# Gates in the gathered rows, and a first mixture that adds its results into a zeroed table

## What is computed

```python
x = _attn_ref(**attn_kwargs).reshape(B * S, D)
# first mixture: logits + log1p(exp(x @ w_noise)) * noise, the two best, softmax over the two
for e in range(E):
    for k in range(2):
        mask = top2[:, k] == e
        h = np.maximum(x[mask] @ w1[e], 0.0)
        out[mask] += top2_w[mask, k, None] * (h @ w2[e])
# second mixture
xn = x / (np.linalg.norm(x, axis=-1, keepdims=True) + 1e-06)
logits = xn @ en.T / tau
expert_idx = np.argmax(logits, axis=1)
gate_w = probs[np.arange(N), expert_idx]
for e in range(E):
    mask = expert_idx == e
    h = np.maximum(x[mask] @ w1[e], 0.0)
    out[mask] = gate_w[mask, None] * (h @ w2[e])
```

## Time and profile before

| | us |
|---|---|
| median of 3 runs | 1224.87 (1224.33 to 1225.34) |
| the profiled execution | 1223.82 |
| its span in the profile | 1222.1 |
| PE busy in the span | 1095.9 |

### The profile page before, as it was taken

How to read it: one execution, slowest core, us unless ns; L and a number is a source line. 1 busy time by engine, 2 the same in 40 slices (tenths; PEclk the granted TensorE clock), 3 DMA queues, 4 the chain that set the end, 5 groups by cost and what they waited for, 6 DMA issues and landing times.

```text
span 1222.1 us, 27227 instructions
## 1 busy us (share of the span) xinstructions
PE 1095.9 (90%) x8052; PEld 1039.5 (85%) x8052; DVE 744.1 (61%) x1406; ACT 553.1 (45%) x1552; POOL 523.2 (43%) x639
## 2 busy tenths in 40 slices
PE   1989188999999999999999999786389999999997
PEld 0556176999999999999999999765279999999997
DVE  8998795446464644646455465386854664466663
ACT  2222285445454544545444454355644554455552
POOL 5887002444444444444444444400324444444444
PEclk9999589999999999999999999988589999999999
DMA  9111201213131121313113111182622313124521
GB/s 325 70 63 52 73 1 42 77 42 99 39 101 42 55 83 40 98 40 101 43 39 93 39 41 41 38 268 92 240 62 64 98 42 100 39 65 125 138 61 35
DMA packets 51188, 97.89 MB, mean 80 GB/s; under 512 B 9651, under 2 KB 33051, under 8 KB 50876
## 3 DMA queue, kind: packets, MB, share of 16 engines
q1 hardware_dynamic: 33084, 61.77, 16.7%
q0 software_dynamic: 18048, 35.42, 10.1%
HBM read 69.62 MB, written 29.10 MB: 81 GB/s over the span
## 4 chain that ended last, share of the span: by engine, by line
PE 78%; DVE 12%; issue 3%; POOL 3%; ACT 2%; DMA 2%; DVEq 0%; POOLq 0%; ACTq 0%; SPq 0%
PE banks L624 22%; PE banks L626 11%; PE banks L610 9%; PE banks L616 7%; PE banks L615 7%; PE banks L611 7%; PE banks L612 7%; DVE prods L889 3%; POOL prods L443 2%; PE banks L586 2%; PE banks L594 2%; PE banks L595 2%; PE banks L550 1%; DVE choices L1092 1%; PE banks L540 1%
## 5 line engine op out<-in xcount | busy, mean ns | idle before, releaser
L1050 DVE SCALAR_TENSOR_TENSOR h_lo<-banks,h_hi 128x256 fp32r<-128x256 f32 x736 | 312.1, 424 | 372.4 <-ACT h_hi L774 315.0
L774 ACT ACTIVATE h_hi<-banks 128x256 fp32r<-128x256 f32 x736 | 283.3, 385 | 448.7 <-PE banks L616 347.6
L624 PE MATMUL banks<-w_hl,h_hi 128*128 128x384 f32 x1472 | 466.0, 353 | 0.0
L626 PE MATMUL banks<-w_hl,h_lo 128*128 128x192 f32 x1472 | 371.1, 252 | 0.0
L626 PEld LDWEIGHTS banks<-w_hl,h_lo 128*128 128x128 f32 x1472 | 279.6, 190 | 0.0
L624 PEld LDWEIGHTS banks<-w_hl,h_hi 128*128 128x128 f32 x1472 | 276.0, 188 | 0.4
L451 POOL DMA_INDIRECT x_slots<-token_rows,gather_idx x192 | 192.4, 1002 | 105.4 <-POOL gather_idx L448 76.2
L610 PE MATMUL banks<-x_hi_a,w_hi 128*128 (+1 forms) x736 | 225.0, 306 | 1.8 <-DVE x_hl_b L1018 1.7
L611 PE MATMUL banks<-x_hi_a,w_lo 128*128 (+1 forms) x736 | 206.5, 281 | 0.0
L616 PE MATMUL banks<-x_hl_b,w_lo 128*128 (+1 forms) x736 | 206.3, 280 | 0.0
L615 PE MATMUL banks<-x_hl_b,w_hi 128*128 (+1 forms) x736 | 205.8, 280 | 0.0
(11 more groups left out here) (170 smaller groups left out, 1255.3 us busy)
## 6 DMA issues: line engine op xcount, KB each, us to landing
raw<-in_moe_w SPq DMA_DIRECT2D x17, 768.0 KB
choices<-choice_rows SPq DMA_DIRECT2D x28, 384.0 KB, 4.2
raw<-in_moe_w SPq DMA_DIRECT2D x17, 512.0 KB
raw<-in_moe_w SPq DMA_DIRECT2D x34, 256.0 KB
x_halo<-in_x SPq DMA_DIRECT2D x2, 2688.0 KB, 15.1
token_rows<-stage SPq DMA_DIRECT2D x14, 384.0 KB, 2.3
token_rows<-rows SPq DMA_DIRECT2D x14, 384.0 KB, 3.9
x_slots<-token_rows,gather_idx POOLq DMA_INDIRECT x192
```

Source lines behind the costliest of these rows:

```text
L624: mm(y[:, i, 0:2 * D], h_hi[:, c % HBUFS, t], w2_hl[u][:, c, :, :], start=c == 0, stop=False)
L626: ins = mm(y[:, i, 0:D], h_lo[:, c % HBUFS, t], w2_hl[u][:, c, 0, :], start=False, stop=c == FC - 1)
L774: sc.activation(h_hi[:, c % HBUFS, :], banks[:, c % HBANKS, 0:BLOCK], ACT.Relu).then_inc(h_hi_ready[m], 1)
L1050: v.scalar_tensor_tensor(h_lo[:, c % HBUFS, :], banks[:, c % HBANKS, 0:BLOCK], 0.0, h_hi[:, c % HBUFS, :].bitcast(F32), ALU.max, ALU.subtr ...
```

## The change

Rows in memory are 193 numbers wide, the last one the gate of the row (`ROW`). Each attention group is stored twice, once for either choice, and the four gate columns follow from SP when the pair gates are ready (`store_gates`). A gather brings the gate along; POOL copies it into a ring of four blocks (`gate_ring`), and ACT and DVE scale the block's results by it, each 128-row half by itself (`take_half`, `add_half`). The first mixture's scatters add into `token_rows[1]`, which SP has filled with zeros from a piece of `logits` during attention; padding slots are added to 256 spare rows. Between the mixtures SP loads each group once, DVE sums the squares, PE turns and scores without filler products between groups. The scaling of rows by the second gate and their store are gone; two gate columns are stored instead. In `positions` the block table is made after the last one-hot, the totals come from differences of the running sum, `not_after` replaces `before` so that the subtraction of the counts is gone, and the gates are finished inside the one-hot loop. The temperature is folded into the embeddings. SP loads the second expert of the second mixture during the first. At the end of a mixture the last block is stored in halves.

```diff
+            sp.wait_ge(zeros_ready, 1)
+            zeros = logits[:, ZEROS_AT:, :].rearrange("p t e -> p (t e)")[:, 0:ROW].unsqueeze(1)
+            all_rows = token_rows[1].rearrange("(p j) d -> p j d", p=P)
+            sp.dma_start(all_rows, zeros.to_broadcast([P, (N + DUMP_ROWS) // P, ROW])).then_inc(x1_zeroed, 16)
...
-                sp.wait_ge(rows_ready[0], g + 1)
-                sp.dma_start(token_view(token_rows[0])[b, :, jj * GROUP:(jj + 1) * GROUP, :],
-                             stage[g % 2][:]).then_inc(rows_stored[g % 2], 16)
-
-
-            with sp.Fori(1, E) as e:
+                sp.wait_ge(rows_ready, g + 1)
+                for k in range(CHOICES[0]):
+                    sp.dma_start(token_view(token_rows[0][k * N:(k + 1) * N])[b, :, jj * GROUP:(jj + 1) * GROUP, 0:D],
+                                 stage[g % 2][:]).then_inc(rows_stored[g % 2], 16)
+
+            def store_gates(m):
+                for k in range(CHOICES[m]):
+                    for b in range(B):
+                        sp.dma_start(token_view(token_rows[m][k * N:(k + 1) * N])[b, :, :, D:D + 1],
+                                     gate[k][:, b * J:(b + 1) * J].unsqueeze(2), allow_slow_non_contiguous=True).then_inc(gates_stored[m], 16)
...
+            sp.wait_ge(weights_ready, 1)
+            load_expert(w1, w2, 1)
+            sp.wait_ge(gates_ready[0], 1)
+            store_gates(0)
...
+            sp.wait_ge(weights_ready, E + 1)
+            load_expert(v1, v2, 1)
...
-                sp.wait_ge(choices_used, g + 1)
...
-                                 src[b, :, jj * GROUP:(jj + 1) * GROUP, :]).then_inc(choices_in[g % CHOICE_BUFS][k], 16)
...
+                sp.dma_start(rows[:, g * GROUP:(g + 1) * GROUP, :],
+                             token_view(token_rows[1][0:N])[b, :, jj * GROUP:(jj + 1) * GROUP, 0:D]).then_inc(x1_in[g], 16)
+            sp.wait_ge(gates_ready[1], 1)
+            store_gates(1)
...
+                def take_gates(n):
+                    at = n % RING * HALVES
+                    gp.tensor_copy(gate_ring[:, bass.ds(at if isinstance(n, int) else pool.snap(at), HALVES)].unsqueeze(2),
+                                   x_slots[:, :, D:D + 1]).then_inc(gates_taken[m], 1)
...
+                    take_gates(g + 2)
...
+                    pool.wait_ge(gates_taken[m], g + 3)
...
+                        if m == 0:
+                            ins = gp.indirect_dma_start(token_rows[1], at, y_slots[:, u, i, :], None, compute_op=ALU.add)
+                        else:
+                            ins = gp.indirect_dma_start(out, at, y_slots[:, u, i, 0:D], None, bounds_check=N - 1, oob_is_err=False)
+                        ins.then_inc(stored[m], 16)
...
+                        pool.wait_ge(stored[m], g * 32)
+                        pool.sem_inc(y_slots_free[m], 1)
+                        copy_idx()
...
+                        pool.wait_ge(half_ready[m], 1)
+                        store_half(0)
+                        pool.wait_ge(y_ready[m], g + 3)
+                        pool.sem_inc(pool_tick, 1)
+                        store_half(1)
...
-            for g in range(SCALE_ACT, NG):
...
-                                 gate[0][:, tiles].unsqueeze(2).to_broadcast([P, GROUP, D]), ALU.mult).then_inc(pool_gated, 1)
...
+            mixture(0, [(rows_stored[u], 32 * (NG // 2)) for u in range(2)] + [(gates_stored[0], 16 * B * CHOICES[0])])
+            mixture(1, [(gates_stored[1], 16 * B)])
...
-            pe.wait_ge(choices_in[0][0], 16)
-            keep_clock(9)
+            keep_clock(26)
...
-                keep_clock(4)
...
+                    if i == 0:
+                        act.wait_ge(gates_taken[m], g + 1)
...
+                    if last and i == 0:
+                        act.wait_ge(half_done[m], 1)
+                    else:
+                        act.wait_ge(h_used[m], g * FC + (FC + HBUFS))
+                    sc.activation(y_half(parity(act, g), i), y[:, i, D:2 * D], ACT.Copy,
+                                  scale=slot_gate(act, g, i)).then_inc(y_copied[m], 1)
...
+                weigh()
...
-                step(v.tensor_tensor(cum[:], cum[:], counts[:], ALU.subtract))
+                step(v.tensor_tensor_scan(cum[:, 1:], flat, flat, 0.0, ALU.add, ALU.max))
+                first_of_expert, last_of_expert = cum[:, 0:E * T:T], cum[:, T::T]
+                step(v.tensor_tensor(totals[:], last_of_expert, first_of_expert, ALU.subtract))
...
+                step(v.scalar_tensor_tensor(pad_off[:], block_end[:, 0:E], float(BLOCK), first_of_expert, ALU.mult, ALU.subtract))
...
+                    if g == HOT_BUFS:
+                        finish_gates()
...
+                block_table()
...
-                v.tensor_scalar(gather_rows[:, 0:cols], q["id_tok"], 0.0, None, ALU.max).then_inc(ids_ready[m], 1)
-                step(v.tensor_scalar(q["id_pad"], ids, 0.0, float(PAD_ROW), ALU.is_equal, ALU.mult))
+                v.tensor_scalar(gather_rows[:, 0:cols], row, -1.0, 0.0, ALU.add, ALU.max).then_inc(ids_ready[m], 1)
...
-                    dve.wait_ge(y_copied[m], g + 1)
-                    slots = y_half(parity(dve, g))
-                    v.tensor_tensor(slots, y[:, :, 0:D], slots, ALU.add).then_inc(y_ready[m], 1)
+                    dve.wait_ge(y_copied[m], g * HALVES + (HALVES + i + 1))
+                    slots = y_half(parity(dve, g), i)
+                    ins = v.scalar_tensor_tensor(slots, y[:, i, 0:D], slot_gate(dve, g, i), slots, ALU.mult, ALU.add)
...
+            def weigh_pairs():
+                v.tensor_tensor(gate[1][:], best[1][:], best[0][:], ALU.subtract).then_inc(route_ask[0], 1)
+
+            def finish_pairs():
+                dve.wait_ge(route_act[0], 3)
+                step(v.tensor_scalar(gate_sum[:], gate[1][:], 1.0, 1e-9, ALU.add, ALU.add))
+                step(v.reciprocal(gate[0][:], gate_sum[:]))
+                v.tensor_tensor(gate[1][:], gate[1][:], gate[0][:], ALU.mult).then_inc(gates_ready[0], 1)
+
+            positions(0, weigh_pairs, finish_pairs)
...
-                    part = choices[u][:, k, :].rearrange("p (i d) -> p i d", d=D)
-                    v.tensor_tensor(part, part, gate[k][:, bass.ds(g * GROUP, GROUP)].unsqueeze(2).to_broadcast([P, GROUP, D]),
...
-                first, second = (choices[u][:, k, :].rearrange("p (i d) -> p i d", d=D) for k in range(2))
-                v.tensor_tensor(to, first, second, ALU.add).then_inc(rows_ready[1], 1)
...
+            for g in range(NG):
+                dve.wait_ge(x1_in[g], 16)
+                if g > 0:
+                    dve.wait_ge(norms_ready, g)
+                tiles = slice(g * GROUP, (g + 1) * GROUP)
+                step(v.tensor_tensor(square[:], rows[:, tiles, :], rows[:, tiles, :], ALU.mult))
+                v.tensor_reduce(sumsq[:, tiles], square[:], AX.X, ALU.add).then_inc(norms_ready, 1)
...
-            positions(1)
+            scores = logits[:, :, 0:E]
+            pick(0, scores)
...
+            def weigh_best():
+                dve.wait_ge(roots_ready, 1)
+                step(v.tensor_scalar(inv_norm[:], inv_norm[:], 1e-6, None, ALU.add))
+                step(v.reciprocal(inv_norm[:], inv_norm[:]))
+                step(v.tensor_tensor(r["noisy"][:], scores, best[0][:].unsqueeze(2).to_broadcast([P, T, E]), ALU.subtract))
+                v.tensor_tensor(r["noisy"][:], r["noisy"][:], inv_norm[:].unsqueeze(2).to_broadcast([P, T, E]),
+                                ALU.mult).then_inc(route_ask[1], 1)
...
+            def finish_best():
+                dve.wait_ge(route_act[1], 1)
+                step(v.tensor_reduce(gate_sum[:], r["noisy"][:], AX.X, ALU.add))
+                step(v.tensor_scalar(gate_sum[:], gate_sum[:], 1e-9, None, ALU.add))
+                v.reciprocal(gate[0][:], gate_sum[:]).then_inc(gates_ready[1], 1)
```

More of the change, by code:

```diff
@@ L169, in attention_moe_moe @@
         h_lo = sb("h_lo", [P, HBUFS, BLOCK], F32R)
-        y_slots = sb("y_slots", [P, 2, HALVES, D])
-        with ExitStack() as between:
-            choices = [sb(f"choices{u}", [P, 2, GC], F32, between) for u in range(CHOICE_BUFS)]
+        y_slots = sb("y_slots", [P, 2, HALVES, ROW])
         r.update({n: sb(n, [P, T, E]) for n in ("soft_u", "soft_w", "soft_ln", "soft_d")})
@@ L838, in _ @@
             sc.activation(r["noisy"][:], r["noisy"][:], ACT.Exp).then_inc(route_act[1], 1)
-            act.wait_ge(route_ask[1], 2)
-            with act.Fori(0, SCALE_ACT) as g:
-                for i in range(GROUP):
-                    tile = rows[:, bass.ds(g * GROUP + i, 1), :].rearrange("p o d -> p (o d)")
-                    ins = sc.activation(tile, tile, ACT.Copy, scale=gate[0][:, bass.ds(g * GROUP + i, 1)])
-                ins.then_inc(gated, 1)
             hot_rows(1)
@@ L922, in _ @@
             finish_rows(NG - 1)
+            v.memset(cum[:, 0:1], 0.0)
+            step(v.memset(block_end[:, 0:1], 0.0))
             def pick(k, scores):
@@ L998, in positions @@
```

(5 more changed lines are left out.)

251 lines of the change are left out of this document (123 added, 128 removed).

## The result

| | before | after |
|---|---|---|
| median of 5 runs, us | 1225.34 (1224.33 to 1226.58) | 1241.05 (1239.25 to 1241.91, and one at 5901.27) |
| the profiled execution | 1223.82 | 1241.91 |
| its span | 1222.1 | 1240.1 |
| PE busy | 1095.9 | 1112.5 |

The ratio is 1.0123, with an interval of 1.0108 to 1.0138: the changed kernel is slower by 1.2%, 15 to 16 us. Forecast were 1198 and a range of 1186 to 1226. The ratio leaves out the one execution at 5901 us, of which no profile exists and which nothing here explains.

The account below looks back on a forecast made before the run. PE bounds the kernel, busy 90% of the span; gains lie in the stages outside the mixtures. Terms +12.1 -3.5 -2.0 -22.5 -4.5 -7.4 +1.35 -0.3 = -26.8 took span 1222.1 to 1195.3, run time 1198; range 1186 to 1226.

Parts of the forecast that it names:

- 1, attention: Attention: zero table queued ahead of doubled row stores stalls DVE 9.1 us, plus 3 for the clock; sum +12.1 us.
- rival D: Attention: the zero table is dear, stall 30.6 us, time 1219; chance 0.08.
- the +3: Attention: PE idles in DVE's stall, its clock falls and delays the next group; +3 us, between 0 and 5.
- 2, first routing: First routing: steps taken off the path before the one-hots, some put back; net -3.5 us.
- 3, the gate columns: Before each mixture's first gather: POOL's new wait for the gate stores is covered; 0 us.
- rival B: Gate columns: each DMA of 4-byte writes costs 18.2 us, POOL's gathers wait; time 1260, slower than before; chance 0.13.
- Rivals A: Gate columns: each DMA of 4-byte writes costs 9.1 us, gates a little late; time 1205; chance 0.14.
- 4, inside the mixtures: Mixtures: gate scaling on ACT and DVE, POOL's gate copies and adding stores all hidden behind PE; 0 us.
- Rival E: Mixtures: adding stores overrun POOL's 2.84 us of slack, by 1 us per block; time 1258; chance 0.03.
- 5, the ends: End of each mixture: half a block stored early; -2.0 us at the kernel's end, -1.3 in the middle.
- 6, scoring: Scoring between the mixtures: PE paces at full clock, 2.2 us per group; cumulated -22.5 us, including the middle's -1.3.
- 7, second routing: Second routing: norm scaling, exp and POOL's row scaling leave the path; -4.5 and -7.4, with +1.35 and -0.3 us.

Follow-up runs that it names:

- e5: Against the changed kernel, the first mixture's stores overwrite instead of adding, so a token keeps only the last stored result; span 1238.7 us against 1240.1.
- e2: Against the changed kernel, the zeroed table of the first mixture's sums has rows of 256 numbers (1024 bytes) instead of 193; span 1231.8 us against 1240.1.
- e4: Against the changed kernel, four filler matmuls added behind the transposes of each scoring group, the 26 ahead of the loop kept; span 1231.4 us against 1240.1.
- e6: Against the changed kernel, the zeroed table has rows of 208 numbers (832 bytes) instead of 193; span 1224.1 us against 1240.1.

## Why the prediction was wrong

**1, attention: the mechanism right, the term mis-sized.** The order of the queue, the buffer that DVE waits for and the share of the clock were as told. The price of a piece was not: I took 394 per us from the load of w2 and called it the only row of that packet size. It is, but those pieces are reads of 768 bytes at a pitch of 768; mine were writes of 772, of which one in sixteen starts on a multiple of 64 bytes, at 242 per us. 7424/242 = 30.7 us for 18.8, which is 11.9 of the 17.5 us that the stall came out longer. The first group's two row stores, at 230 pieces per us, are 4.5 us for 2.6, another 1.9. The 3.7 us that are left lie between the end of the table and the landing of those stores; no run splits them further. The bound that I had set above, half the w2 rate (rival D, stall 30.6), holds the 26.6, and I gave it 8 in 100. What came on top of the stall was 3.4 us against the +3.

**2, first routing:** -3.8 for -3.5. Right.

**3, the gate columns:** nothing, as forecast, and with room. In 192 to 200 us 5945 packets under 512 bytes passed in the changed kernel, 743 per us:

```profile
DMA packets 5946, 0.04 MB, mean 5 GB/s; under 512 B 5945, under 2 KB 5945, under 8 KB 5945
```

A DMA of 3,584 elements is then 4.8 us and not 6.6; over all four, 14,400 packets from about 185 to 206 us, it was 5.2. To outweigh the gain, as in rival B, 12.4 would have been needed. Rivals A and B fall: of 4-byte writes the engines pass three times as many per us as of 772-byte ones. The Trainium skill, "DMA: Bandwidth & Descriptors", Specifications, puts the least piece for the line rate at 512 bytes, with a read-modify-write below it. In bytes the trace agrees, 743 pieces of 4 bytes being 3 GB/s against the 187 of the table's; whether anything was read back no run shows, and it cost this kernel no time.

**4, inside the mixtures:** 0.6 us for 0. Right; POOL's stores grew by 0.61 us each (1.62 for 1.02, 0.63 above e5's) and stayed under its slack. Rival E falls.

**5, the ends: the step failed.** I let half of the last block go early. But POOL first waits until the stores of the block before have landed, in the middle (815.95, released by a DMA) as at the kernel's end (1233.41):

```profile
1233.41 0.18 POOL L495 COPY store_idx<-store_rows 128x2 int32 x1 [1.63 <-DMA out_rows<-y_slots,store_idx]
1234.49 0.98 POOL L501 DMA_INDIRECT out_rows<-y_slots,store_idx  x1 [0.90 <-DVE y_slots L1106]
```

In the middle that landing, not the half block, is last. At the kernel's end it comes about when the half block is ready (DVE's two halves run from 1233.01 to 1233.78), but the index copy stands behind that wait and so does not come early. From the last product to the end of the span it took 8.1 us for 8.8: 0.7 of the 2.0 us came, and 0.4 of that the second mixture gave back. In the middle the loss of 2.9 us splits by the timeline: the first store starts 4.10 us behind the last product instead of 3.13 (+1.0), two adding issues are 1.1 longer, and SP's first load follows the last issue by 2.08 instead of 1.22 (+0.9). Two blocks may add to one token's row, so I take the wait to be needed for adding stores; no run went without it. The step to see was in the diff: wait_ge(stored[m], g * 32) stands ahead of everything of the last block.

**6, scoring: the step that failed was the clock.** "PE runs 26 filler matmuls meanwhile and is then dense, so I take the full clock." PE was dense and at half. The 2.2 us per group were the right price at the full clock: the first two scores in e2, where the clock was up again for a moment, came 2.00 us apart. At 0.50 a group took 3.73. I had written the price of the other case beside it, up to 31 us, and it was 21; but I gave it no chance of its own among the rivals, and so a dear table together with a fallen clock, which is what happened, was not in the range: 1198 + 17.5 (a stall of 26.6 for 9.1) + 21 + 6 (both ends) gives about 1242. The row that should have warned was in the earlier trace rows: in the second routing PE was busy 14.21 of 19.00 us and stood at 0.50. And the change removed four wide products from each group of a loop whose others are transposes and products of 16 columns.

**7, second routing:** -11.1 for -10.85. Right: the long steps of 8 elements are gone with POOL's scaling, 0.17 us each in the trace of after.

```profile
886.29 0.17 DVE L1006 TENSOR_SCALAR totals_i<-totals_i 128x8 int32<-128x8 int32 x1
```

Of the rivals none was the cause by itself. D names the cause of 18 of the 45 us between forecast and measurement; the 21 of the fallen clock stood in no rival.

## What to carry to other kernels

Put a large store that nobody waits for soon behind the small ones that a buffer waits for, and work out its time from the pieces as they will lie in memory: a row widened by one number, from 192 to 193, leaves the multiples of 64 bytes, and a piece cost 66 ns of an engine where one of a row padded to 208 cost 40. Before filler products are taken out of a loop, ask what the rest of it does to the clock; try the number of fillers, since below the one that holds the level each is only a cost. And when two risks of a forecast are each priced, give their coincidence a case of its own.

## What the runs showed of the hardware

- Writes to HBM by full DMA engines: 242 pieces per us of 772 bytes at a pitch of 772, 230 of 768 at 772, 399 of 832 at 832, 378 of 1024 at 1024, 743 of 4 bytes (192 to 200 us). Those of 1024 carry 387 GB/s, those of 772 carry 187.
- An adding indirect store of 128 rows issues in 1.62 us and takes 3.6 us from issue to landing; a plain one issues in 1.0. Of the first the page of its tile says:

```profile
DMA to landing us min/median/max: 3.5/3.6/8.4
```

- PE busy in all of 24 us of records stood at 0.50 in the loop of transposes and 16-column products, with none, one or two 128x512 bf16 products for every 18 others; with three or four it stood at 1.00. It also rose from 0.50 to 1.00 in that loop, with four (e4), where it stayed, and with none (e2), where it fell again though PE was busy throughout.
- In e2, e6 and the changed kernel PE, never waiting and at full clock, passed 776, 786 and 783 matmuls per 100 us in the same mixture. That stays open.
